# Where a sorted-token buffer gets its zero rows: first rows of every expert during attention, or behind each expert's last token

## The chip, the cores and the metric

One core of a Trainium2 chip runs the whole program. The metric is the device time of one execution in microseconds (us). The kernel before takes 522.28 us, the median of three runs (520.22 to 523.31).

## The reference

Block-summary attention gives 1536 token rows of 512 values. Each row goes through one of eight experts (top-1 by a gate), and the result goes through a dense network with a squared ReLU.

```python
x = attn_out.transpose(0, 2, 1, 3).reshape(1536, 512)
logits = x @ w_gate + modality_bias[modality_id]
e_idx = np.argmax(logits, axis=1)          # one of 8 experts per token
...
for e in range(8):
    mask = e_idx == e
    if not mask.any(): continue
    h = np.maximum(x[mask] @ w1[e], 0.0)       # 512 -> 1024
    out[mask] = gate_w[mask, None] * (h @ w2[e])   # 1024 -> 512
...
h = np.maximum(out @ w_in, 0.0)            # 512 -> 2048
return h * h @ w_out                       # 2048 -> 512
```

## The kernel before, in words

The work has three stages. **Attention** runs in NB = 12 steps of P = 128 tokens. SP loads the queries and values of each step, POOL builds the keys, TensorE (PE) computes scores, transposes and values, ACT the exponentials, DVE maxima and normalisation. The result of a step stands in `X[:, i, :]`; PE then computes its gate logits, and DVE routes the tokens in the five groups of `RGROUPS`.

**Sorting** goes through DRAM. `xs_d` has 128 rows at its start and behind them a section of EROWS = 1536 rows for each of the E = 8 experts. POOL scatters token rows into it with indirect DMAs (`scatter(g)`, L785 to L790): the token with rank r of expert e goes to row 128 + EROWS e + r. How many tokens an expert has (`cnt`) is known when the last group is routed (L925).

**Experts** are computed in tiles of 128 rows that are read back from `xs_d` into two buffers `x_in`. An expert's last tile is its last 128 rows, so it overlaps the tile before, but an expert with fewer than 128 tokens has a tile that reaches beyond its last token. Those rows must hold finite numbers, and zeros are put there. The kernel does it before the counts are known: from step i = ZFIRST = 5 of SP's load loop (L465 to L475) one DMA of 256 KB fills rows 0 to 127 of `xs_d`, and four DMAs of 512 KB fill the first 128 rows of two sections each, 2.36 MB in five DMAs on SP's queue. POOL waits for all five (L804) before the first scatter, which may overwrite them.

The most common expert so far is chosen early, and the first tiles are its: tiles 0 and 1 are loaded by POOL (L809 to L811), tile 2 by SP (L496). For tile 3 and on the rows come out of a table that DVE works out from the counts (L1142 to L1199, the last write is T_ROW, semaphore `rows`). SP waits for `rows` (L497) and then for x_t (a transpose that frees the buffer) and issues `load_x(3)` and `load_x(4)` (L486 to L488); each loads a register from the table in SBUF, computes the address and issues a DMA. On PE the order is written out: layer 1 of tile 2, the first six eighths of layer 2 of tile 1, the transposes of tile 3 (L1600, L1492), the rest of layer 2. PE runs its instructions in order, so it stands still if tile 3 has not landed. DVE's order is written out too: the last weight split (L1136), lsub (L1140), the tables, `x_low(2)` (L1168), which layer 1 of tile 2 waits for, more tables, `h_low(1)`, which layer 2 of tile 1 waits for.

Weights of the second expert come in two 2 MB DMAs that POOL issues (L849): the first after the semaphore `slots` (L1167), the second once tile 3 has landed (L867). `Seq` (L357, here `r`) is a helper on DVE: each instruction raises a semaphore and the next one waits for it.

After the experts comes the **dense network**, in which PE has dense work from L1653 to L1670.

Of the kernel before, what the change touches and what calls it, by code (L numbers as in the profile page):

```python
# [5 lines left out]
F32 = mybir.dt.float32  # L6
# [4 lines left out]
ALU = mybir.AluOpType  # L11
# [3 lines left out]
P = 128  # L15
# [7 lines left out]
NBS = S // P  # L23
# [12 lines left out]
N, DM, E, FE = B * S, H * D, 8, 1024  # L36
KD = DM // P
KF = FE // P
SPEC = 3
TILES = (N + E * (P - 1)) // P + SPEC - 1  # L40
EROWS = N
LEAST = N // P
RECENT = 4
WE = KD * FE
# [19 lines left out]
T_NR = T_DONE + 1  # L64
T_E0 = T_NR + 1
T_X0 = T_E0 + 1
T_ALL = T_X0 + SPEC

AHEAD = 1
VPITCH = 9 * P  # L70
# [6 lines left out]
TRI = 4  # L77
SPLIT_AHEAD = PARTS - 1
EARLY = 1
ZFIRST, ZSTEP = NBS - 1, 2  # L80
FRAC = 16


# [16 lines left out]
def constants():  # L100
# [4 lines left out]
    def put(a, table, name, v):  # L105
        lo, hi = table[name]
        a[:, lo:hi] = v
# [5 lines left out]
    put(f, CF, "tile_row", P * np.arange(TILES + 1)[None])  # L113
    put(f, CF, "base", (EROWS * np.arange(E) + P)[None])
    put(f, CF, "run", np.arange(E)[None])
# [7 lines left out]
    first = np.zeros((P, E), np.float32)  # L123
    first[0] = EROWS * np.arange(E) + P
    assert (first == first.astype(np.dtype("bfloat16"))).all()
# [19 lines left out]
def build(nc, a):  # L145

    base = (nc.sbuf_base + 63) // 64 * 64
# [5 lines left out]
    def sb(region, name, shape, dt):  # L153
        n = size[dt] * int(np.prod(shape[1:]))
        n = (n + 31) // 32 * 32
        t = nc.alloc_sbuf_tensor_at(name, shape, dt, offset=cursor[region])
        cursor[region] += n
        assert cursor[region] <= end[region], (name, cursor[region] - end[region])
        return t
# [5 lines left out]
    sorted_m = sb("c", "sorted_m", [P, NB + GT, 2], F32)  # L165
    table = sb("c", "table", [P, T_ALL], I32)
    waited = sb("c", "waited", [P, 4], F32)
# [3 lines left out]
    zero = sb("c", "zero", [P, DM], F32)  # L171
# [49 lines left out]
    spec_c = sb("t", "spec_c", [P, 2], F32)  # L221
    least = sb("t", "least", [P, E], F32)
    skip = sb("t", "skip", [P, E], F32)
    tiles = sb("t", "tiles", [P, E], F32)
    real = sb("t", "real", [P, E], F32)
    begin = sb("t", "begin", [P, 3, E + 1], F32)
# [20 lines left out]
    cnt = sb("t", "cnt", [P, E], F32)  # L247
# [51 lines left out]

    xs_d = nc.dram_tensor("xs_d", (P + E * EROWS, DM), F32).ap()  # L300
    ys_d = nc.dram_tensor("ys_d", (N + P, DM), F32).ap()
    meta_d = nc.dram_tensor("meta_d", (N, 2), F32).ap()

    def cfv(name):
        lo, hi = CF[name]
        at = CF["thr"][0]
        return cr[:, lo - at:hi - at]
# [5 lines left out]
    def wide(ap, axis, n):  # L313

        u = ap.unsqueeze(axis)
        shape = list(u.shape)
        shape[axis] = n
        return u.broadcast_to(shape)

    def Wv(slot, lo, col, n):  # L320
# [7 lines left out]
    names = """const const_r ident w_gate mbias cleared zero ones bias_ok logit rk  # L328
        ksum kw sc mx ex tr0 tr1 pt0 pt1 pv norm xt xtc lg rank oneh rowd vtsum sums vm vsum
        meta metas sorted rows placed slots rout oh tab n_run e0 x0 warm early lsub scat_b scat_c scat_d x2  # L330
        raw0 raw1 zfill scat_a x_t x_h x_l l1 relu ht hh hl l2 y sh sla slbv slbp
        counts both ylast wo_h wo_v zin scale zt zh zl m1 r sqs s_h s_l mo o_a o_v out ofree den_ok""".split()
    sem = {n: nc.alloc_semaphore("s_" + n) for n in names}
    s_q = [nc.alloc_semaphore(f"s_q{s}") for s in range(RING)]
# [5 lines left out]
    s_x0 = [nc.alloc_semaphore(f"s_x0_{t}") for t in range(2)]  # L340
# [72 lines left out]
    with block:  # L413

        @block.sync
        def _(sp):
            def load_q(i):
                if i >= RING:
                    sp.wait_ge(sem["sc"], i - RING + 1)
                sp.dma_start(q_in[i % RING][:, :, :], a["q"][i]).then_inc(s_q[i % RING], 16)  # L420

            def load_v(i):
                if i >= VRING:
                    sp.wait_ge(sem["pv"], i - VRING + 1)
                sp.dma_start(v_in[i % VRING][NSUM:KEYS, :, :, :].rearrange("p a h d -> p (a h d)"), a["v"][i, :, 0:2 * H * (D + 1)]).then_inc(s_v[i % VRING], 16)
# [16 lines left out]
            def load_weights(e, part):  # L442
                for n in (part, part + 1):
                    w, k = (w1_v, KD // PARTS) if n < PARTS else (w2_v, KF // PARTS)
                    j = n % PARTS
                    sp.dma_start(raw[:, n * PW:(n + 1) * PW].rearrange("p (k f) -> p k f", k=k),
                                 w[bass.ds(e, 1), :, j * k:(j + 1) * k, :].rearrange("a p k f -> (a p) k f")
                                 ).then_inc(s_raw0[n], 16)
# [16 lines left out]
            for i in range(VRING, NB):  # L465
                load_v(i)
                if i + RING < NB:
                    load_q(i + RING)
                if i == ZFIRST:
                    sp.wait_ge(sem["zero"], 1)  # L470
                    sp.dma_start(xs_d[0:P, :], zero[:, :]).then_inc(sem["zfill"], 16)
                if ZFIRST <= i < ZFIRST + E // ZSTEP:
                    some = slice((i - ZFIRST) * ZSTEP, (i - ZFIRST + 1) * ZSTEP)
                    sp.dma_start(xs_d[P:, :].rearrange("(e r) d -> r e d", e=E)[0:P, some], wide(zero[:, :], 1, ZSTEP)
                                 ).then_inc(sem["zfill"], 16)  # L475
                if i == NB - RING:
                    sp.wait_ge(sem["e0"], 1)
                    e = sp.value_load(table[0:1, T_E0:T_E0 + 1], min_val=0, max_val=E - 1)
                    load_weights(e, 0)
# [6 lines left out]
            def load_x(t, s):  # L486
                row = sp.value_load(table[0:1, bass.ds(t + T_ROW, 1)], min_val=0, max_val=E * EROWS)
                sp.dma_start(x_in[s][:, :], xs_d[bass.ds(row, P), :]).then_inc(s_xs[s], 16)  # L488
# [3 lines left out]
            sp.wait_ge(sem["x2"], 1)  # L492
            row = sp.value_load(table[0:1, T_X0 + 2:T_X0 + 3], min_val=0, max_val=E * EROWS)
            sp.wait_ge(sem["scat_d"], RGROUPS[4][1] * 16)
            sp.wait_ge(sem["x_t"], 1)
            sp.dma_start(x_in[0][:, :], xs_d[bass.ds(row, P), :]).then_inc(s_xs[0], 16)  # L496
            sp.wait_ge(sem["rows"], 1)  # L497

            def moe_step(t, s):
                sp.wait_ge(sem["x_t"], t)  # L500
                load_x(t + 1, 1 - s)
# [5 lines left out]
            with sp.Fori(0, (TILES - SPEC) // 2) as m:  # L507
                t = m * 2 + SPEC
# [242 lines left out]
        def _(pool):  # L751
# [33 lines left out]
            def scatter(g):  # L785

                pool.wait_ge(sem["rowd"], g + 1)
                for i in range(RGROUPS[g][0], sum(RGROUPS[g])):
                    pool.indirect_dma_start(out=xs_d, out_offset=bass.IndirectOffsetOnAxis(ap=dest[:, i:i + 1], axis=0),
                                            in_=X[:, i, :], in_offset=None).then_inc(sem["scat_" + "aabcd"[g]], 16)  # L790
# [10 lines left out]
            sums_of(NBS + 2)  # L801
            sums_of(NBS + 3)

            pool.wait_ge(sem["zfill"], (1 + E // ZSTEP) * 16)  # L804
            scatter(0)
            scatter(1)
            pool.wait_ge(sem["scat_a"], sum(RGROUPS[SETTLED - 1]) * 16)
            pool.wait_ge(sem["x0"], 1)
            for t in range(2):  # L809
                row = pool.value_load(table[0:1, T_X0 + t:T_X0 + t + 1], min_val=0, max_val=(E - 1) * EROWS + 2 * P)  # L810
                pool.dma_start(x_in[t][:, :], xs_d[bass.ds(row, P), :]).then_inc(s_x0[t], 16)  # L811
# [89 lines left out]
        def _(dve):  # L901
# [74 lines left out]
            r = Seq(dve, sem["rout"])  # L976
# [160 lines left out]

            dve.tensor_tensor(lsub[:, :, :], logit[:, :, :], wide(lmax[:, :], 2, E), ALU.subtract).then_inc(sem["lsub"], 1)  # L1140
            T1 = TILES + 1
            r(dve.tensor_scalar(used[:, :], cnt[:, :], 0.0, None, ALU.is_gt))  # L1142
# [157 lines left out]
            with dve.Fori(0, (TILES - SPEC) // 2) as m:  # L1300
                t = m * 2 + SPEC
# [18 lines left out]
            with dve.Fori(0, GROUPS) as g:  # L1320
                for f in range(KFF):
                    n = g * KFF + f
# [401 lines left out]
```

## Time and profile before

| What | Value |
|---|---|
| Median of three runs | 522.28 us |
| The profiled execution's own time | 521.77 us |
| Its span, first to last instruction | 520.1 us |
| PE busy (matmul) | 508.1 us, 98% of the span |
| PE weight load busy | 410.0 us, 79% |
| DVE, ACT, POOL busy | 225.4, 188.0, 87.1 us |
| Granted TensorE clock | 0.998 of full speed |
| DMA | 54.92 MB, mean 106 GB/s |

The 1.67 us between span and own time lie outside the instructions. The DMA engines are used unevenly: nearly fully over the first 52 us, in bursts of weights up to about 250 us, and hardly after.

### The profile page before, as it was taken

Reading aid. Unit: us, or ns where it says so; the run is one execution under the profiler, and the core shown is the slowest. Engines: PE = TensorE matmul, PEld = TensorE weight load, DVE = VectorE, ACT = ScalarE, POOL = GpSimd, SP = SyncE. Lnnn points to the kernel's source line nnn. Section 1 sums busy time; section 2 is a strip of 40 time slices with the busy share of each in tenths; the row PEclk is TensorE's granted clock in tenths of the full one; section 3 lists DMA queues with packets and bytes.
Section 4 is the critical chain, followed back from the end, with each engine's and each line's share of the span. In section 5 each row is a group of like instructions: output and inputs, shape, how many; then the busy total and the mean of one; then the engine's idle time right before and its main releaser. Section 6 shows DMA issues by size and latency. Waiting matters only on the chain.

```text
span 520.1 us, 9415 instructions
## 1 busy us (share of the span) xinstructions
PE 508.1 (98%) x3115; PEld 410.0 (79%) x3117; DVE 225.4 (43%) x440; ACT 188.0 (36%) x355; POOL 87.1 (17%) x110
## 2 busy tenths in 40 slices
PE   8889999999999999999999999999999999999995
PEld 3678788888888888888788888888888888888884
DVE  4787686974323554237632422342242233222221
ACT  1876665243524544225522212331221233122121
POOL 4434335027600223100000000300000020000002
PEclk9999999999999999999999999999999999999999
DMA  8999666384661655521200000400000020000002
GB/s 285 336 290 340 235 220 228 99 285 104 189 216 41 219 204 202 202 82 40 83 1 1 0 1 0 161 0 0 0 0 0 0 81 0 0 0 0 0 0 81
DMA packets 19018, 54.92 MB, mean 106 GB/s; under 512 B 2848, under 2 KB 3120, under 8 KB 18480
## 3 DMA queue, kind: packets, MB, share of 16 engines
q1 hardware_dynamic: 11200, 27.47, 16.6%
q0 software_dynamic: 5200, 23.62, 12.6%
q10 hardware_dynamic: 2592, 3.49, 1.8%
q8 instruction: 15, 0.25, 0.2%
q14 instruction: 11, 0.09, 0.1%
HBM read 42.51 MB, written 12.07 MB: 105 GB/s over the span
## 4 chain that ended last, share of the span: by engine, by line
PE 95%; DVE 3%; issue 1%; ACT 1%; POOL 0%; POOLq 0%; DVEq 0%; ACTq 0%
PE psum L1653 9%; PE psum L1654 9%; PE psum L1652 9%; PE psum L1668 8%; PE psum L1669 8%; PE psum L1670 8%; PE psum L1536 5%; PE psum L1559 5%; PE psum L1538 5%; PE psum L1560 5%; PE psum L1561 5%; PE psum L1537 5%; PE psum L1396 2%; PE psum L1569 2%; PE psum L1371 2%; PE psum L1456 2%
## 5 line engine op out<-in xcount | busy, mean ns | idle before, releaser
L1326 DVE TENSOR_TENSOR sq<-r_sb 128x512 f32<-128x512 f32 x48 | 33.2, 692 | 141.4 <-ACT r_sb L734 137.4
L734 ACT ACTIVATE r_sb<-psum 128x512 f32<-128x512 f32 x48 | 28.7, 597 | 143.7 <-PE psum L1654 143.7
L1668 PE MATMUL psum<-W,s_hi 128*128 128x512 f32 x192 | 75.9, 395 | 0.1
L1653 PE MATMUL psum<-z_lo,W 128*128 128x512 f32 x192 | 75.8, 395 | 0.0
L1654 PE MATMUL psum<-z_hi,W 128*128 128x512 f32 x192 | 75.8, 395 | 0.0
L1652 PE MATMUL psum<-z_hi,W 128*128 128x512 f32 x192 | 75.8, 395 | 0.0
L1669 PE MATMUL psum<-W,s_hi 128*128 128x512 f32 x192 | 75.5, 393 | 0.0
L1670 PE MATMUL psum<-W,s_lo 128*128 128x512 f32 x192 | 75.4, 393 | 0.0
L893 POOL DMA_INDIRECT out<-o_sb,sorted_m x12 | 11.6, 969 | 293.5 <-DVE o_sb L1342 291.6
L1328 DVE TENSOR_TENSOR s_lo<-sq,s_hi 128x512 fp32r<-128x512 f32 x48 | 33.2, 692 | 33.5 <-ACT s_hi L736 33.5
L736 ACT ACTIVATE s_hi<-sq 128x512 fp32r<-128x512 f32 x48 | 30.3, 632 | 41.8 <-DVE sq L1326 41.8
L1668 PEld LDWEIGHTS psum<-W,s_hi 128*128 128x128 f32 x192 | 36.1, 188 | 8.7 <-issue 0.5
L1652 PEld LDWEIGHTS psum<-z_hi,W 128*128 128x128 f32 x192 | 36.0, 188 | 8.7
L1654 PEld LDWEIGHTS psum<-z_hi,W 128*128 128x128 f32 x192 | 36.0, 187 | 8.7
L1653 PEld LDWEIGHTS psum<-z_lo,W 128*128 128x128 f32 x192 | 36.0, 188 | 8.6
L1670 PEld LDWEIGHTS psum<-W,s_lo 128*128 128x128 f32 x192 | 36.1, 188 | 8.2
L1669 PEld LDWEIGHTS psum<-W,s_hi 128*128 128x128 f32 x192 | 36.1, 188 | 8.1
L1536 PE MATMUL psum<-W,x_hi 128*128 (+1 forms) x104 | 42.1, 405 | 0.3 <-DVE x_lo L1018 0.3
L1559 PE MATMUL psum<-W,h_hi 128*128 (+1 forms) x104 | 42.0, 404 | 0.0
L1538 PE MATMUL psum<-W,x_lo 128*128 (+1 forms) x104 | 40.9, 393 | 0.0
L1560 PE MATMUL psum<-W,h_hi 128*128 (+1 forms) x104 | 40.9, 393 | 0.0
L1561 PE MATMUL psum<-W,h_lo 128*128 (+1 forms) x104 | 40.7, 391 | 0.0
(205 smaller groups left out, 729.5 us busy)
## 6 DMA issues: line engine op xcount, KB each, us to landing
raw<-in_w POOLq DMA_DIRECT2D x4, 2048.0 KB, 9.1
raw<-in_w_io POOLq DMA_DIRECT2D x4, 2048.0 KB, 8.2
v_in<-in_v SPq DMA_DIRECT2D x12, 390.0 KB, 12.7
raw<-in_w SPq DMA_DIRECT2D x8, 512.0 KB, 4.3
kT<-in_kT SPq DMA_DIRECT2D x8, 400.0 KB, 7.9
q_in<-in_q SPq DMA_DIRECT2D x12, 256.0 KB, 8.8
X<-in_vT SPq DMA_DIRECT2D x4, 768.0 KB, 11.7
x_in<-xs_d SPq DMA_DIRECT2D x12, 256.0 KB, 2.8
```

The costliest lines, as they stand in the source:

```text
L1326: dve.tensor_tensor(sq[:, :], r_sb[:, :], r_sb[:, :], ALU.mult).then_inc(sem["sqs"], 1)
L1536: pe.matmul(bank[h][:, :], x_hi[:, k, :], wh, start=(k == 0), stop=False)
L1538: ins = pe.matmul(bank[h][:, :], x_lo[:, k, :], wh, start=False, stop=(k == KD - 1))
L1559: pe.matmul(bank[4][:, :], h_of(t)[1][:, k, :], wh, start=(k == 0), stop=False)
L1560: pe.matmul(bank[4][:, :], h_of(t)[1][:, k, :], wl, start=False, stop=False)
L1561: ins = pe.matmul(bank[4][:, :], h_lo[:, k, :], wh, start=False, stop=(k == KF - 1))
L1652: pe.matmul(bank[f % 2][:, :], wh, z_hi[:, k, :], start=(k == 0), stop=False)
L1653: pe.matmul(bank[f % 2][:, :], wh, z_lo[:, k, :], start=False, stop=False)
L1654: ins = pe.matmul(bank[f % 2][:, :], wl, z_hi[:, k, :], start=False, stop=(k == KD - 1))
L1668: pe.matmul(bank[2 + j][:, :], s_hi[f % SBUFS][:, tok], wh, start=(f == 0), stop=False)
L1669: pe.matmul(bank[2 + j][:, :], s_hi[f % SBUFS][:, tok], wl, start=False, stop=False)
L1670: ins = pe.matmul(bank[2 + j][:, :], s_lo[f % SBUFS][:, tok], wh, start=False, stop=(f == KFF - 1))
```

## The change

The five zero DMAs become one (rows 0 to 127 only). A section grows by 128 rows, EROWS = 1664, so that each has 128 spare rows at its end. DVE computes, once `cnt` is there, one row per expert into new table entries: the row behind its last token if it has fewer than 128 tokens, and otherwise the spare rows. SP loads each of the eight into a register and issues eight DMAs of 256 KB (2.10 MB) there; then it waits for their completion before it goes on to `load_x(3)`. POOL's wait for the zero DMA (now 16, not 80) moves from before scatter(0) to behind scatter(1).

```diff
-EROWS = N
+EROWS = N + P
@@ tables
-T_ALL = T_X0 + SPEC
+T_PAD = T_X0 + SPEC
+T_ALL = T_PAD + E
-ZFIRST, ZSTEP = NBS - 1, 2
+ZFIRST = NBS - 1
@@ SP, load loop
                 if i == ZFIRST:
                     sp.wait_ge(sem["zero"], 1)
                     sp.dma_start(xs_d[0:P, :], zero[:, :]).then_inc(sem["zfill"], 16)
-                if ZFIRST <= i < ZFIRST + E // ZSTEP:
-                    some = slice((i - ZFIRST) * ZSTEP, (i - ZFIRST + 1) * ZSTEP)
-                    sp.dma_start(xs_d[P:, :].rearrange("(e r) d -> r e d", e=E)[0:P, some], wide(zero[:, :], 1, ZSTEP)
-                                 ).then_inc(sem["zfill"], 16)
@@ SP, behind the load of tile 2
             sp.dma_start(x_in[0][:, :], xs_d[bass.ds(row, P), :]).then_inc(s_xs[0], 16)
+            sp.wait_ge(sem["pads"], 1)
+            for t in range(2):
+                sp.wait_ge(s_x0[t], 16)
+            for n in range(E):
+                pad = sp.value_load(table[0:1, T_PAD + n:T_PAD + n + 1], min_val=P, max_val=E * EROWS)
+                sp.dma_start(xs_d[bass.ds(pad, P), :], zero[:, :]).then_inc(sem["zpad"], 16)
             sp.wait_ge(sem["rows"], 1)
+            sp.wait_ge(sem["zpad"], E * 16)
@@ POOL
-            pool.wait_ge(sem["zfill"], (1 + E // ZSTEP) * 16)
             scatter(0)
             scatter(1)
+            pool.wait_ge(sem["zfill"], 16)
             pool.wait_ge(sem["scat_a"], sum(RGROUPS[SETTLED - 1]) * 16)
@@ DVE, before lsub (L1140)
+            r(dve.tensor_scalar(pad_f[:, 0, :], cnt[:, :], float(P), float(N), ALU.is_ge, ALU.mult))
+            r(dve.tensor_tensor(pad_f[:, 1, :], pad_f[:, 0, :], cnt[:, :], ALU.max))
+            dve.tensor_tensor(table[:, T_PAD:T_PAD + E], pad_f[:, 1, :], cfv("base"), ALU.add).then_inc(sem["pads"], 1)
             dve.tensor_tensor(lsub[:, :, :], logit[:, :, :], wide(lmax[:, :], 2, E), ALU.subtract).then_inc(sem["lsub"], 1)
```

## Rows read from the trace of the kernel before

**Rows 1.** The page: busy time of each engine (share, instructions); chain that ended last.

```profile
PE 508.1 (98%) x3115; PEld 410.0 (79%) x3117; DVE 225.4 (43%) x440; ACT 188.0 (36%) x355; POOL 87.1 (17%) x110
...
PE 95%; DVE 3%; issue 1%; ACT 1%; POOL 0%; POOLq 0%; DVEq 0%; ACTq 0%
```

**Rows 2.** SP's timeline: start us, us, engine, line, operation, tiles; attention.

```profile
31.09 0.43 SPq L471 DMA_DIRECT2D xs_d<-zero  x1
...
47.66 0.43 SPq L474 DMA_DIRECT2D xs_d<-zero  x1
```

**Rows 3.** Stretches of attention: length, busy (instructions) per engine, PEclk, DMA share, GB/s.

```profile
38.00:47.00 9.00, 8.84 (x152) 7.52 (x151) 5.79 (x16) 6.41 (x20) 1.29 (x3) 1.00 1.03 374
47.00:52.00 5.00, 5.00 (x98) 4.10 (x87) 4.29 (x14) 3.59 (x11) 4.68 (x6) 1.00 0.87 283
```

**Rows 4.** PE's timeline, attention; in brackets the idle time before and its releaser.

```profile
36.07 1.03 PE L1396 MATMUL psum<-v_in,pT 120*64 120x65 f32 x26
38.16 0.39 PE L1396 MATMUL psum<-v_in,pT 120*64 120x65 f32 x6 [1.06 <-issue]
```

**Rows 5.** DMA queues, 35-36 us (two), 38-39 us: packets, MB, share.

```profile
q1 hardware_dynamic: 75, 0.24, 94.8%
q8 instruction: 1, 0.02, 7.9%
...
q1 hardware_dynamic: 179, 0.37, 103.1%
```

**Rows 6.** POOL's timeline, the first scatter.

```profile
53.02 1.17 POOL L789 DMA_INDIRECT xs_d<-X,dest  x1 [1.34 <-DMA xs_d<-zero]
```

**Rows 7.** DVE's timeline from the last weight split to the row table.

```profile
93.25 0.25 DVE L1140 TENSOR_TENSOR lsub<-logit,lmax 128x96 f32<-128x96 f32 x1
...
97.64 0.17 DVE L1167 CAST table<-exp_f 128x8 int32<-128x8 f32 x1
97.72 0.68 DVE L1018 TENSOR_TENSOR x_lo<-psum,x_hi 128x512 fp32r<-128x512 f32 x1
...
98.92 0.17 DVE L1173 TENSOR_SCALAR beyond<-cnt 128x8 f32<-128x8 f32 x1
99.12 0.17 DVE L1174 TENSOR_TENSOR per_e<-beyond,cr 128x8 f32<-128x8 f32 x1
...
103.31 0.18 DVE L1199 CAST table<-row_t 128x22 int32<-128x22 f32 x1
```

**Rows 8.** PE's timeline: layer 1 of tile 2, weight loads of tile 3's transposes.

```profile
98.46 0.50 PE L1536 MATMUL psum<-W,x_hi 128*128 128x512 f32 x1
...
108.40 0.42 PEld L1492 LDWEIGHTS psum<-ident,x_in 128*128 128x128 f32 x4 [0.31 <-DMA x_in<-xs_d]
```

**Rows 9.** SP's timeline: the loads of tiles 3 and 4.

```profile
104.24 0.35 SPq L488 DMA_DIRECT2D x_in<-xs_d  x1
...
105.37 0.34 SPq L488 DMA_DIRECT2D x_in<-xs_d  x1
```

**Rows 10.** DMA issues: size, us to landing; last row 100 to 109 us.

```profile
raw<-in_w POOLq DMA_DIRECT2D x4, 2048.0 KB, 9.1
...
x_in<-xs_d SPq DMA_DIRECT2D x12, 256.0 KB, 2.8
...
ys_d<-y_last SPq DMA_DIRECT2D x1, 256.0 KB, 2.1
...
x_in<-xs_d SPq DMA_DIRECT2D x2, 256.0 KB, 4.1
```

**Rows 11.** Landing time of the last zero write, issued at 47.66 us.

```profile
DMA to landing us min/median/max: 5.1/5.1/5.1
```

**Rows 12.** POOL's and ACT's timeline: second expert's weights loaded and first used.

```profile
99.13 0.81 POOL L849 DMA_DIRECT2D raw<-in_w  x1 [4.08 <-issue]
...
114.48 3.90 ACT L585 ACTIVATE W<-raw 128x1024 fp32r<-128x1024 f32 x4 [2.47 <-DVE y_sb L1179]
```

**Rows 13.** A stretch beside this load, columns as in rows 3.

```profile
104.00:105.00 1.00, 1.00 (x6) 0.74 (x5) 0.96 (x4) 0.00 (x0) 0.00 (x0) 1.00 1.06 438
```

More of the change, by code:

```diff
@@ L223, in build @@
     skip = sb("t", "skip", [P, E], F32)
+    pad_f = sb("t", "pad_f", [P, 2, E], F32)
     tiles = sb("t", "tiles", [P, E], F32)
@@ L330, in build @@
         meta metas sorted rows placed slots rout oh tab n_run e0 x0 warm early lsub scat_b scat_c scat_d x2
-        raw0 raw1 zfill scat_a x_t x_h x_l l1 relu ht hh hl l2 y sh sla slbv slbp
+        raw0 raw1 zfill pads zpad scat_a x_t x_h x_l l1 relu ht hh hl l2 y sh sla slbv slbp
         counts both ylast wo_h wo_v zin scale zt zh zl m1 r sqs s_h s_l mo o_a o_v out ofree den_ok""".split()
```

## The prediction

> **What bounds the kernel now.** I read the page first: PE is busy for 98% of the span and makes 95% of the chain that ended last [rows 1]. So two things alone can move the time: PE idle time that goes away, and PE idle time that is new. I then looked at the two places that the change touches. The first is attention, where the zero writes are issued from 31.09 to 47.66 us [rows 2]. From 38 to 47 us the DMA engines are saturated (share 1.03, 374 GB/s), which looks like a bottleneck, but PE is busy for 8.84 of 9.00 us there, and for 5.00 of 5.00 us from 47 to 52 [rows 3]. The reader is to see that a full DMA column beside a full PE column says that nobody waits for the DMAs. The second place is the start of the expert stage, 93 to 109 us, read engine by engine in time order. There PE's only idle time is 0.31 us at 108.40, before the transposes of tile 3, and the releaser is the load of `x_in` [rows 8]. That small row matters most: the load of tile 3 has no slack at all now, and the change puts four waits and eight DMAs in front of it on SP.
>
> **Part 1, zero writes leave attention.** Removed are four DMAs of 512 KB, 2.10 MB, at some 370 GB/s 5.7 us of DMA time [rows 3]. Who waits for them? POOL alone: 1.34 us before the first scatter at 53.02 [rows 6]. What it waited for on PE's side comes much later (tile 0), and scatter 1 waits for DVE's routing of its group (L787) whenever scatter 0 starts; so this gives PE nothing. The one PE idle time nearby is 1.06 us from 37.10 on (36.07 + 1.03) [rows 4]. It is inside a run of 32 like matmuls (after 26), so no semaphore ends it. Could the zero writes cause it? At 35 to 36 us SP's queue moves 75 packets for 0.24 MB, 3.2 KB each; at 38 to 39 us 179 for 0.37 MB, 2.07 KB each, the size of one row of `xs_d` [rows 5]. The queue is worked off in order, so the zeros issued at 31.09 seem to flow from about 37.5 only, behind a backlog of values and keys that stays. I take 0 us of gain, with 1.06 us as the bound; a loss is excluded as nothing is added in this stage. SP is past five issues of about 0.43 us earlier (now one), and the loads queued behind them come earlier, but PE waits for none of these.
>
> **Part 2, three small DVE instructions before lsub.** Two are chained by `r`, whose period for 8 elements is 0.20 us (98.92 to 99.12), the third is followed by an instruction that doesn't wait for it, 0.08 us (97.64 to 97.72) [rows 7]. Sum 0.20 + 0.20 + 0.08 = 0.48 us. What is behind it on DVE: `x_low(2)` ends at 97.72 + 0.68 = 98.40 and layer 1 of tile 2 starts at 98.46 [rows 7, 8]. There is no cover worth the name, so PE moves by 0.4 to 0.5 us, and the row table (end 103.31 + 0.18 = 103.49) by the same.
>
> **Part 3, eight pads on SP.** The pad rows are in the table at 93.25 + 0.20 + 0.20 + 0.17 = 93.82 us [rows 7]. SP is free by then, as tile 2, which PE uses ahead of tile 3, has been issued, and the waits on tiles 0 and 1 are long fulfilled. How long from the release to a DMA with an address from the table? The row table ends at 103.49 and load_x(3) starts at 104.24, 0.75 us. How long is the period? load_x(3) to load_x(4), the same sequence plus a wait that is already fulfilled, 105.37 - 104.24 = 1.13 us [rows 9]. So the first pad is issued at 94.57 and the eighth at 94.57 + 7 x 1.13 = 102.5 us. The first six have the DMA engines nearly to themselves: 0.26 MB each 1.13 us is 232 GB/s, against 370 and more shown [rows 3]. The last two meet the weights, which POOL issues at 99.13 (now 99.6) and which fill the engines at 104 (438 GB/s) [rows 12, 13]. Landing of a 256 KB write: 2.1 us with nothing beside it; of a 256 KB load beside the weights 4.1 us, where the median of all takes 2.8 [rows 10], so 1.3 us for the company, and 2.1 + 1.3 = 3.4 us for the last pad: 105.9 us. The other bound is the last 512 KB zero write, 5.1 us [rows 11]. I take 3.4, the same size and the same company.
>
> Then SP wakes (the wait on `rows`, 103.97, is already behind it), loads the register and issues load_x(3) at 105.9 + 0.75 = 106.65 us, 2.4 us later than 104.24. Its landing should be shorter than 4.1 us: 2.1 MB of weights, issued at 99.6 and flowing from about a microsecond later, plus the two late pads (0.5 MB) end about 107.5 at 0.39 MB/us (between the 374 of rows 3 and the 438 GB/s of rows 13), just as its data start. I take 3.3 us, between 2.8 and 4.1. So tile 3 lands at 109.95 and the transposes start at 110.0 instead of 108.40, **+1.6 us**. The 0.48 us of DVE don't add to it: both are waits of the same PE stream, and PE comes to this place at 108.4 - 0.3 + 0.48 = 108.6 and stands for another 1.4 us. Nothing behind it gives the time back, as PE runs on without idle time. Bounds: with 2.1 us for the last pad (104.6) and 2.8 for the load, tile 3 lands at 108.15 and only DVE's 0.5 us are left. With 5.1 us for the pad (107.6), 0.75 and 4.1, it lands at 112.45: +4.1 us.
>
> **Who waits behind it.** The second half of the weights is issued by POOL when tile 3 has landed (L867) and is then 1.6 us later. The first half lands at 99.13 + 9.1 = 108.2 and, with 0.48 us of DVE and 0.5 MB of pads at 0.39 MB/us ahead of it, 1.8 us later, at 110.0; its first user is ACT at 114.48 [rows 10, 12]. That is 4.5 us of cover, so it costs nothing; without the cover it would be up to 1.8 us more.
>
> A rule of the Trainium skill bears on part 3: "DMA: Bandwidth & Descriptors", section "Anatomy of one DMA — SWDGE (gpsimd) path", says that a DMA costs a fixed 2.0 us plus its bytes at 436 GB/s, most of the fixed part being the receipt of the write, longest where the target is HBM; every pad is such a write, and SP waits for its receipt. By that rule an estimate for 256 KB is 2.6 us, the last pad would land at 105.1 and the loss be 0.8 us; the trace has 2.1 us for such a write in quiet, so the rule is roughly borne out, but it has no term for the weights beside it.
>
> **The rivals.**
> (a) *The pads are hidden*: they land before the row table and only DVE's instructions are paid. For it: SP has 10 us between 93.8 and 103.97, and 2.1 MB need only 5.7. Against it: the issue period of 1.13 us, not the bandwidth, sets the pace. +0.5 us, 522.8. Chance 0.17.
> (b) *The weights hold the pads up*: slower by over 0.5%. From about 100.8 us on the last two or three pads share the engines with 2 MB, and the completion that SP waits for comes late. It decides from the point at which tile 3 lands after 111.0 us, that is when the last pad takes over 4.5 us or the period over 1.27 us. At the upper bound +4.1 us, 526.4. For it: 438 GB/s at 104 us. Against: the last pad is small. Chance 0.22.
> (c) *Attention gains*: the stall of 1.06 us is gone as the DMA queues are less full, and the zeros were in its way after all. For it: it falls 6 us after the first zero issue, with the engines saturated, and one 16 KB packet of the instruction queue at 35 us [rows 5] shows that instructions come by DMA too. Against it: the packet sizes. 1.6 - 1.06 = +0.5 us, 522.8; with the pads hidden too 0.5 - 1.06 = -0.6, 521.7. Chance 0.15; a gain of over 2.6 us needs more idle time than attention shows after 31 us, and I give it 0.05 of its own.
> The page "Runtime: NRT & Kernel Launch", section "Instruction fetch mechanics", of the Trainium skill speaks for (c): a sequencer fetches its next 256 instructions with a DMA of its own while it works on the current ones. It calls the cost mostly hidden; the row of 1.06 us shows one that probably isn't.
>
> **How the numbers follow.** The forecast, +1.6 us, has 0.41: 521.77 + 1.6 = 523.4 for the profiled execution (span 521.7), and 0.51 us more for the median, 522.28 + 1.6 = 523.9. The range reaches from (c) with hidden pads, 521.7, to (b), 526.4; the three runs lie 2 us below and 1 us above their median, so I take 520.4 to 526.9. A measurement of this kernel tells 0.5%, 2.6 us, from no change. Slower by that: (b), 0.22, and 0.03 of the forecast's upper part, 0.25. Faster: 0.05. Within: 0.70.
>
> **What would show it.** DVE: x_lo of tile 2 about 0.48 us later against the last weight split. SP: eight zero writes from about 1.3 us after that split, 1.13 us apart; if they are under 0.9 apart, (a). PE: an idle time before L1492 of tile 3 of about 1.4 us, released by `x_in`; over 2.5 us is (b), none is (a). Attention: the 1.06 us stall is there as before, else (c). DMA from 40 to 52 us is well below saturation, with PE as busy as it was. I am wrong if PE's pace in attention changes outside of such a stall, or if new idle time comes anywhere else.

## The result

The changed kernel takes 532.62 us (median of four runs, 530.13 to 535.27) against 521.26 us for the kernel before (520.22 to 523.31): a ratio of 1.0191, 95% interval 1.0147 to 1.0235 (the two medians alone would give 1.0218). It is slower by 10 to 11 us, where +1.6 us was forecast.

The page of the changed kernel: busy times, granted clock in 40 slices, chain that ended last; the busy times and the chain of before are in [rows 1].

```profile
span 533.6 us, 9463 instructions
...
PE 513.9 (96%) x3116; PEld 411.8 (77%) x3117; DVE 226.1 (42%) x443; ACT 187.9 (35%) x355; POOL 86.9 (16%) x110
...
PEclk9998999999999999999999999999999999999999
...
PE 85%; DMA 7%; DVE 2%; SPq 2%; issue 1%; POOLq 0%; POOL 0%; ACT 0%; ACTq 0%
```

PE's share of the chain fell from 95% to 85% and DMA has entered it with 7%. But PE's busy time also rose, from 508.1 to 513.9 us, for the same matmuls: not all of the loss is waiting. The span is 13.5 us longer. A convenient ruler is the start of the transposes of each tile on PE (L1492 before, L1500 after), which cuts the span in parts that can be compared between kernels.

PE's timeline of the changed kernel: transposes of tiles 2, 3 and 4.

```profile
100.23 0.60 PE L1500 MATMUL psum<-ident,x_in 128*128 128x128 f32 x4
...
118.20 0.74 PE L1500 MATMUL psum<-ident,x_in 128*128 128x128 f32 x4 [4.72 <-DMA x_in<-xs_d]
...
128.15 0.60 PE L1500 MATMUL psum<-ident,x_in 128*128 128x128 f32 x4
```

The same in the kernel before: the one of tile 3 follows its weight load at 108.40 [rows 8]; the ones of tiles 2 and 4:

```profile
95.83 0.60 PE L1492 MATMUL psum<-ident,x_in 128*128 128x128 f32 x4
...
116.68 0.60 PE L1492 MATMUL psum<-ident,x_in 128*128 128x128 f32 x4
```

| Part of the span | Before | After | Longer by |
|---|---|---|---|
| start to tile 2 | 95.83 | 100.23 | 4.4 |
| tile 2 to tile 3 | 12.58 | 17.97 | 5.4 |
| tile 3 to tile 4 | 8.27 | 9.95 | 1.7 |
| tile 4 to the end | 403.4 | 405.5 | 2.0 |

Four parts, and the prediction spoke of one. **Tile 2 to 3** is the pads. The fences that follow show SP's timeline (last pad, load of tile 3), SP's wait for the pads, and the landing times of the pads (shortest, median, longest):

```profile
107.38 0.33 SPq L500 DMA_DIRECT2D xs_d<-zero  x1
...
115.50 0.36 SPq L486 DMA_DIRECT2D x_in<-xs_d  x1
```

```profile
SPq L505 <- DMA xs_d<-zero: 7.0, 1, 7.0
```

```profile
DMA to landing us min/median/max: 2.0/2.1/7.4
```

The pads go out 1.1 us apart, as forecast, but for the last, which follows after 1.47 us. The first five land in 2.0 to 2.1 us. The last three, issued at 104.8, 105.9 and 107.4, take 6.3, 7.2 and 7.4 us. POOL issued the weights at 104.03. What the queues did from 106 to 108 us, then from 108 to 110 (q0: POOL's, q1: SP's; packets, MB, share):

```profile
q0 software_dynamic: 97, 0.40, 77.9%
q1 hardware_dynamic: 4, 0.01, 1.1%
...
q0 software_dynamic: 137, 0.56, 71.5%
q1 hardware_dynamic: 115, 0.23, 29.7%
```

SP's queue moved 4 packets from 106 to 108 us while two pads, and from 107.4 on three, had been issued and had not landed. So SP waits 7.0 us, and the load of tile 3 leaves 15.27 us after the start of tile 2's transposes (115.50 - 100.23); in the kernel before [rows 9] it was 8.41 us (104.24 - 95.83).

**Tile 3 to 4** is the clock. PE stood still for 4.72 us; right behind it (stretches of 1 us; the number before the DMA share is the granted clock):

```profile
118.00:119.00 1.00, 0.80 (x5) 0.80 (x6) 0.00 (x0) 0.02 (x1) 0.00 (x0) 0.82 0.83 221
119.00:120.00 1.00, 1.00 (x3) 0.74 (x3) 0.32 (x1) 0.58 (x1) 0.56 (x1) 0.50 0.09 33
120.00:121.00 1.00, 1.00 (x4) 0.78 (x3) 0.37 (x1) 0.00 (x0) 0.38 (x1) 0.50 0.39 41
121.00:122.00 1.00, 1.00 (x6) 0.80 (x5) 0.66 (x3) 0.00 (x0) 0.00 (x0) 0.50 0.94 274
122.00:123.00 1.00, 1.00 (x8) 0.93 (x7) 0.83 (x6) 0.69 (x2) 0.00 (x0) 0.97 1.02 180
```

From 119 to 122 us the clock is 0.50, the 1.2 GHz level, and PE, full as it looks, has 3 and then 4 matmuls in a microsecond, where it has 6 at full clock [rows 13]. The other two parts don't point at the change. **The last** has no idle time at all. **The first** is longer before any line that the change touches, and it has a stretch at the lower clock of its own, from 43.5 to 47 us, behind a stop of PE of 2.33 us; the kernel before has none in attention:

```profile
44.00:45.00 1.00, 1.00 (x7) 0.22 (x11) 0.98 (x3) 0.78 (x2) 0.00 (x0) 0.50 0.85 207
```

These two were the first thing to test.

### The profile page after: what moved, and what is told of

Read it like the earlier page. It is cut to its first block, busy times and chain, and to the rows that moved or that the text cites. A ratio compares the mean times of both kernels' runs of the same rounds, so it can differ in the third digit from the quotient of the medians.

```text
span 533.6 us, 9463 instructions
## 1 busy us (share of the span) xinstructions
PE 513.9 (96%) x3116; PEld 411.8 (77%) x3117; DVE 226.1 (42%) x443; ACT 187.9 (35%) x355; POOL 86.9 (16%) x110
## 4 chain that ended last, share of the span: by engine, by line
PE 85%; DMA 7%; DVE 2%; SPq 2%; issue 1%; POOLq 0%; POOL 0%; ACT 0%; ACTq 0%
PE psum L1661 8%; PE psum L1660 8%; PE psum L1662 8%; PE psum L1676 8%; PE psum L1677 8%; PE psum L1678 8%; DMA X<-in_vT 6%; PE psum L1567 4%; PE psum L1568 4%; PE psum L1569 4%; PE psum L1544 4%; PE psum L1545 4%; PE psum L1546 4%; PE psum L1577 2%; PE psum L1419 2%; PE psum L1404 2%
## 5 line engine op out<-in xcount | busy, mean ns | idle before, releaser
L1678 PE MATMUL psum<-W,s_lo 128*128 128x512 f32 x192 | 75.5, 393 | 0.0
L1567 PE MATMUL psum<-W,h_hi 128*128 (+1 forms) x104 | 42.8, 411 | 0.1
L1568 PE MATMUL psum<-W,h_hi 128*128 (+1 forms) x104 | 41.5, 399 | 0.0
```

Source lines behind the costliest of these rows:

```text
L1567: pe.matmul(bank[4][:, :], h_of(t)[1][:, k, :], wh, start=(k == 0), stop=False)
L1568: pe.matmul(bank[4][:, :], h_of(t)[1][:, k, :], wl, start=False, stop=False)
L1678: ins = pe.matmul(bank[2 + j][:, :], s_lo[f % SBUFS][:, tok], wh, start=False, stop=(f == KFF - 1))
```

## The experiments

**The changed kernel again, and the two halves of the change in attention.** First the unchanged "after" for a second profile; then the longer sections alone; then the missing zero writes alone; then the changed kernel with the wait on the pads behind the loads of tiles 3 and 4.

> The changed kernel again, for a second profile. In the first one three things made the loss: 4.3 us until the last weight split (input loads of attention late by 1 to 4 us, which began before any line that the change touches), 5.4 us of waiting for tile 3, 1.7 us at half clock behind it. If the attention part belongs to the change, it is there again (3 us or more). If it is the luck of one execution or of one chip, it is under 1.5 us against the kernel before on this chip, and the total loss falls to 6 to 8 us. The wait for tile 3 (4 to 6 us) should stand in both cases.

Measured: 532.47 us, ratio 1.0222 (1.0143 to 1.03). Tile 2 is at 95.38 us, 0.5 us earlier than before, so the 4.4 us of attention are gone; tile 2 to 3 is 17.79 us (+5.2), tile 3 to 4 10.65 (+2.4), the rest +2.7:

```profile
113.17 1.12 PE L1500 MATMUL psum<-ident,x_in 128*128 128x128 f32 x4 [4.55 <-DMA x_in<-xs_d]
```

The three later parts belong to the change, the first to the execution. (Of the last part, some 0.6 us is one tile step of 13.21 us with a stop of PE of 0.45 us in it, which the first profile doesn't have.) The fall of the total to 6 to 8 us that I expected with it did not come.

```diff
-EROWS = N
+EROWS = N + P
```

> The kernel before with nothing changed but the length of a section, 1664 for 1536 rows. Theory layout (longer sections move what lies in DRAM, and with it the pace of the input loads): slower by 3 to 5 us, all of it in attention, as in the changed kernel. Theory luck: within 1 us of the kernel before. Theory emptier queue (it is the missing zero writes that harm attention in some way): within 1 us as well.

Measured: 522.53 us, ratio 0.9989 (0.9958 to 1.002). Longer sections cost nothing.

```diff
@@ SP, load loop
-                if ZFIRST <= i < ZFIRST + E // ZSTEP:
-                    some = slice((i - ZFIRST) * ZSTEP, (i - ZFIRST + 1) * ZSTEP)
-                    sp.dma_start(xs_d[P:, :].rearrange(...)[0:P, some], wide(zero[:, :], 1, ZSTEP)).then_inc(sem["zfill"], 16)
+                    sp.dma_start(xs_d[P + 3 * EROWS:2 * P + 3 * EROWS, :], zero[:, :]).then_inc(sem["zfill"], 16)
@@ POOL
-            pool.wait_ge(sem["zfill"], (1 + E // ZSTEP) * 16)
+            pool.wait_ge(sem["zfill"], 2 * 16)
```

> The kernel before with one zero write of 256 KB in attention in place of the four of 512 KB (only the section that has under 128 tokens in this data; the other sections' zeros are left out), nothing else. It is the first half of the change alone. My prediction: no gain, within 1 us. Rival: the stalls of PE in attention go with the DMA traffic, 1 to 1.5 us faster. Theory emptier queue: 3 us or more slower.

Measured: 523.06 us, ratio 1.0016 (0.9991 to 1.0042). No gain, as forecast. The start of tile 0's transposes tells the same over all profiles of this study: in the ten with four zero writes in attention it lies between 71.97 and 76.59 us (mean 73.5), in the eight without between 71.80 and 76.77 (mean 74.2). Attention's length varies by 5 us from one execution to the next, whatever the kernel. What goes with it is the clock: in five of the 18 profiles (two with the four writes, three without) the granted clock is 0.50 for 3.4 us somewhere between 41 and 61 us, and these are the five latest, 75.5 to 76.8 us; the thirteen with a full clock there lie between 71.8 and 74.8 us.

```diff
             sp.wait_ge(sem["rows"], 1)
-            sp.wait_ge(sem["zpad"], E * 16)
...
             moe_step(3, 1)
+            sp.wait_ge(sem["zpad"], E * 16)
             sp.wait_ge(sem["counts"], 1)
```

> The changed kernel, but SP waits for the eight pads only after the loads of tiles 3 and 4, which in this data don't read pad rows. If the wait is what costs (7 us in the first profile: 5.4 us of waiting and 1.7 us of half clock), the kernel is 5 to 7 us faster than the changed one and the wait before tile 3 is under 1 us. Rival: it is the traffic of pads and weights itself that makes tile 3 late, as the load now stands behind the pads in the same queue; then PE still waits 3 us or more.

Measured: 529.68 us, ratio 1.011 (1.006 to 1.016), only 2.8 us faster than the changed kernel beside it; the wait of PE is 1.63 us. Neither was right: SP's wait for the pads is most of PE's stop (4.55 to 1.63 us), but not all. From tile 2 on this profile is 5.8 us shorter than that of the changed kernel, twice what the medians show; it has the low clock in attention instead, and of its four runs the one with the highest granted clock (0.997) took 527.08 us, the other three (0.994 and 0.995) 529.7 to 529.8. SP issues the load of tile 3 at 108.29, as early as it could wish, and that load itself takes 5.9 us to land, behind late pads and beside the weights. There was no half clock behind it: tile 3 to 4 took 8.36 us. And the last part was still 2.2 us longer, with neither waiting nor a low clock in front of it.

**The part without idle time.** In every profile with pads so far a tile took 12.51 us and not 12.34 (the time from one tile's transposes to the next one's). The pads' table entries are the one thing left that PE can feel: `table` is eight words longer, and all buffers behind it in SBUF move. In the kernel before they start 1216 bytes behind the region's begin, now 1248.

```diff
-T_ALL = T_X0 + SPEC
+T_PAD = T_X0 + SPEC
+T_ALL = T_PAD + E
```

> The kernel before with its table eight words longer and nothing else. In all three profiles of kernels with pads each expert tile behind tile 4 takes 12.51 us and not 12.34, and the time from tile 4 to the end is 2.0 to 2.7 us longer, with no idle time on PE; the kernels without pads don't show it. The longer table moves all buffers behind it in SBUF by 32 bytes, from 19 x 64 to 19.5 x 64 bytes. Theory addresses: this kernel shows 12.51 us as well and is 2 to 2.7 us slower than the kernel before. Rival (traffic, or later timing of the weights): 12.34 us and no loss.

Measured: 524.54 us, ratio 1.0073 (1.0038 to 1.0108). Two of its tiles in PE's timeline, then the same two of the kernel before:

```profile
141.24 0.60 PE L1493 MATMUL psum<-ident,x_in 128*128 128x128 f32 x4
153.75 0.60 PE L1493 MATMUL psum<-ident,x_in 128*128 128x128 f32 x4
```

```profile
153.98 0.60 PE L1492 MATMUL psum<-ident,x_in 128*128 128x128 f32 x4
166.32 0.60 PE L1492 MATMUL psum<-ident,x_in 128*128 128x128 f32 x4
```

12.51 us against 12.34, and tile 4 to the end +2.1 us, with no pad, no wait and not one instruction more. An unused table entry costs what looked like work.

```diff
-T_ALL = T_PAD + E
+T_ALL = T_PAD + 2 * E
```

> The changed kernel with a table that is another eight words longer, so that the buffers behind it lie at a multiple of 64 bytes again. Theory addresses: a tile takes 12.34 us, the kernel is 2 to 2.7 us faster than the changed one (about 530 us), and the wait for tile 3 of 4.5 us stays. Rival: 12.51 us, 532.5 us.

Measured: 521.66 us, ratio 1.0002 (0.998 to 1.0023), 11 us less than the changed kernel, where 2 to 2.7 were expected. The wait for tile 3 is still 4.58 us and the clock still falls; but a group of the dense network (from the transposes of its second group of 512 tokens to those of the third) takes 89.00 us, where the kernel before had 90.96. The direction was right, the size not: 1280 bytes is no return to the old place but a better one.

**The parts of the pads, at 1280 bytes.** The DVE instructions alone, put ahead of lsub in the kernel before:

```diff
+            r(dve.tensor_scalar(pad_f[:, 0, :], cnt[:, :], float(P), float(N), ALU.is_ge, ALU.mult))
+            r(dve.tensor_tensor(pad_f[:, 1, :], pad_f[:, 0, :], cnt[:, :], ALU.max))
+            dve.tensor_tensor(table[:, T_PAD:T_PAD + E], pad_f[:, 1, :], cfv("base"), ALU.add).then_inc(sem["pads"], 1)
```

> The kernel before with the three DVE instructions that compute the pad rows, buffers at a multiple of 64 bytes, no pads on SP. My prediction for this part: +0.48 us, tile 2's transposes to tile 3's 12.58 + 0.48 = 13.06 us. Rival: DVE has slack after all, 12.58 us and no loss.

Measured: 516.78 us, ratio 0.992 (0.9892 to 0.9948); tile 2 to 3 12.90 us. I had compared with the wrong place: beside the kernel before at 1280 bytes (12.42 us, below) it is exactly 0.48 us.

The changed kernel at 1280 bytes, where POOL holds the weights until the pads have landed:

```diff
             pool.wait_ge(sem["slots"], 1)
+            pool.wait_ge(sem["zpad"], E * 16)
             load_w(1, 0)
```

> The changed kernel, aligned as before, and POOL waits until the eight pads have landed before it issues the second expert's first weights. Theory weights (the last two pads stand beside the weights and so take up to 7.4 us to land): every pad lands in 2.0 to 2.2 us, PE waits under 0.7 us for tile 3, no half clock follows, 523 to 524.5 us. Rival (the issue pace of 1.1 us a pad and the register loads are what makes tile 3 late): PE still waits 2 us or more. A loss of its own would show if the weights, 4 us later, reach ACT too late.

Measured: 516.91 us, ratio 0.9927 (0.9898 to 0.9956); the 523 to 524.5 us expected were for the place at 1216 bytes. All eight pads land in 2.0 to 2.2 us, SP's wait for them is 1.7 us and PE doesn't wait for tile 3 at all; ACT waits 5.1 us for the later weights, which PE doesn't notice. Pads' landing, and SP's wait:

```profile
DMA to landing us min/median/max: 2.0/2.0/2.2
```

```profile
SPq L505 <- DMA xs_d<-zero: 1.7, 1, 1.7
```

One wait on POOL takes 4.7 us of the changed kernel away (521.66 to 516.91 us), and with it the low clock. That settles the weights as the cause of the late pads.

The kernel before at 1280 bytes, the table 16 words longer and nothing else:

```diff
-T_ALL = T_X0 + SPEC
+T_PAD = T_X0 + SPEC
+T_ALL = T_PAD + 2 * E
```

> The kernel before with its table 16 words longer, so that the buffers behind it in SBUF start at 1280 bytes (10 x 128) and not at 1216 (9.5 x 128). The kernel with the three DVE instructions at 1280 took 516.8 us, a tile 12.29 us, a group of the dense network 89.0 and not 90.97 us. Theory 128 bytes: all of this gain is the address; this kernel takes 516.4 us, and tile 2's to tile 3's transposes take 12.4 us, 0.48 us less than the 12.90 with the DVE instructions. Rival (the DVE instructions cost nothing or help in some way): 516.8 us or more, 12.9 us.

Measured: 515.49 us, ratio 0.9851 (0.9809 to 0.9892); a tile takes 12.26 us, a group 89.03, tile 2 to 3 12.42. It is faster than both kernels of this case. The whole price of the change at a good place is 521.66 - 515.49 = 6.2 us; these medians come from two chips, and from tile 2 on the two profiles differ by 7.5 us.

One pad in place of eight:

```diff
-            for n in range(E):
+            for n in (3,):
...
-            sp.wait_ge(sem["zpad"], E * 16)
+            sp.wait_ge(sem["zpad"], 16)
```

> The changed kernel at 1280 bytes with one pad in place of eight, that of the one expert with under 128 tokens (the other seven are left out). Theory weights: this pad lands in 2.1 us, long before the row table; no wait for tile 3 beyond 0.5 us, no half clock; 516.8 us, as with the DVE instructions alone. Rival (the wait or the register load on SP cost something themselves): over 518 us.

Measured: 518.72 us, ratio 0.9911 (0.9878 to 0.9944). PE doesn't wait for tile 3. The total is 1.9 us above the expected one; with 518.72 the number of the rival (over 518 us) was met, though not its mechanism: from tile 2 to tile 3 it is 13.09 us, 0.2 more than with the DVE instructions alone. The profile shows a PE wait of 1.16 us two tiles later, released by DVE's x_lo; other profiles have one of 0.2 to 0.5 us before the same line (layer 1), in one tile each. Whether its length belongs to the pad or to this execution stays open.

Seven of the eight pads cut to 16 rows:

```diff
+                if n == 3:
+                    sp.dma_start(xs_d[bass.ds(pad, P), :], zero[:, :]).then_inc(sem["zpad"], 16)
+                else:
+                    sp.dma_start(xs_d[bass.ds(pad, 16), :], zero[0:16, :]).then_inc(sem["zpad"], 16)
```

> The changed kernel at 1280 bytes; eight pads at the same pace, but seven of them (all but the one that is needed) write 16 rows and not 128, 32 KB. Theory bytes: the three pads issued after the weights are late since their 128 KB each and more get a small share beside 2 MB; with an eighth they land in 2 to 3 us and PE waits under 0.7 us for tile 3 (516.8 to 517.5 us). Rival (whatever is issued on SP's queue once the weights run is held up, however small): they land in 5 us or more and PE still waits 2.5 us or more (519 us or more).

(The "128 KB" in it should read 256 KB, the size of a pad.) Measured: 520.14 us, ratio 0.9939 (0.9909 to 0.997). The landing times of the small ones, and PE's wait for tile 3:

```profile
DMA to landing us min/median/max: 1.6/1.6/5.2
```

```profile
113.82 0.66 PE L1503 MATMUL psum<-ident,x_in 128*128 128x128 f32 x4 [2.02 <-DMA x_in<-xs_d]
```

An eighth of the bytes does not help in proportion: a write of 32 KB that takes 1.6 us alone takes up to 5.2 us beside the weights' start. PE's wait of 2.0 us lies between the two expectations, the landing time and the total are the rival's; most of the hold-up is being queued at that time, not the size. No half clock follows this stop either: tile 3 to 4 is 8.23 us.

**Which place is good, and for whom.** The kernel before with a table 32, 48 and 80 words longer (the edit is that of the experiments above, with 4 * E, 6 * E and 10 * E):

> The kernel before with its table 32 words longer: buffers behind it from 1344 bytes, 10.5 x 128, a multiple of 64 but not of 128, as 1216. Theory 128 bytes: a tile takes 12.34 us and the kernel 521 to 523 us, as before. Rival (the place of the buffers as such, or anything else at 1280): 12.29 us and 516 to 517 us.

Measured: 525.2 us, ratio 1.0036 (1.0012 to 1.0059). Neither expectation: 1344 bytes is worse than 1216.

> The kernel before with a table 48 words longer: buffers behind it from 1408 bytes, 11 x 128. At 1344 (10.5 x 128) a tile took 12.52 and a group 90.71 us, at 1216 (9.5 x 128) 12.34 and 90.97, so multiples of 64 that are none of 128 are not all alike. Theory 128 bytes: as at 1280, 12.29 us, 89.0 us, 515.5 us. Theory 256 bytes (1280 is 5 x 256, 1408 is 5.5 x 256): 12.4 us or more a tile, 90 us or more a group, 520 us or more.

Measured: 523.93 us, ratio 1.0037 (1.0005 to 1.0069). A multiple of 128 is not enough.

> The kernel before with a table 80 words longer: buffers behind it from 1536 bytes, 6 x 256. Theory 256 bytes (1280 is the one good place among 1216, 1248, 1280, 1344 and 1408, and the one multiple of 256): a tile takes 12.3 us, a group 89.0 us, the kernel 515.5 us. Rival (1280 is good for another reason): 12.4 to 12.5 us, 90.5 us or more, 521 us or more.

Measured: 515.22 us, ratio 0.987 (0.9813 to 0.9927), as the theory of 256 bytes had it.

| Buffers start at | A tile | A group of the dense network | Median |
|---|---|---|---|
| 1216 (kernel before) | 12.34 | 90.96 | 521 to 523 |
| 1248 (changed kernel's place) | 12.51 | 91.20 | 524.54 |
| 1280 = 5 x 256 | 12.26 | 89.03 | 515.49 |
| 1344 | 12.52 | 90.71 | 525.20 |
| 1408 = 11 x 128 | 12.50 | 91.07 | 523.93 |
| 1536 = 6 x 256 | 12.26 | 89.02 | 515.22 |

Then, at 1216, two sets of buffers by themselves 64 bytes further on: those of the up projection (`cursor["c"] = after_moe + 64`), and those of the down projection (`cursor["c"] = c_mark + 64` ahead of `z_in`).

> The kernel before with only the buffers z_part, z_hi and z_lo 64 bytes further on (a multiple of 128), all others where they were. The address gain at 1280 bytes has two parts, 3 x 2 us in the dense network (a group 90.97 to 89.0 us) and 0.05 us a tile. Theory z: the moving operand of the up projection sets it, a group takes 89.0 to 89.3 us and the kernel 516 to 517 us. Theory s: nothing here, 91 us. Both: about 90 us.

Measured: 517.05 us, ratio 0.99 (0.9871 to 0.9929), a group 89.37 us: theory z.

> The kernel before with only z_in, r_sb, sq, s_hi, s_lo and o_sb of the dense network 64 bytes further on. Theory s: the stationary operand of the down projection (or what ACT and DVE write for it) sets it, a group takes 89.0 to 89.3 us. Theory z: 91 us. Both: about 90 us.

Measured: 520.51 us, ratio 0.9984 (0.9959 to 1.001), a group 90.57 us. The two effects, 1.6 and 0.4 us a group, add up to the gain of 1.9 us at 1280 bytes. Matmuls from 340 to 400 us: the up projection (z) and the down projection (s) of the kernel before, then of the first of these two.

```profile
L1652 PE MATMUL psum<-z_hi,W 128*128 128x512 f32 x43 | 17.0, 395 | 0.0
L1670 PE MATMUL psum<-W,s_lo 128*128 128x512 f32 x43 | 16.9, 393 | 0.0
```

```profile
L1652 PE MATMUL psum<-z_hi,W 128*128 128x512 f32 x47 | 18.3, 389 | 0.0
L1670 PE MATMUL psum<-W,s_lo 128*128 128x512 f32 x41 | 15.9, 388 | 0.0
```

The place of the up projection's buffers decides most of it, and `z_hi` and `z_lo`, which stream through PE there, are the likely ones: 395 ns a matmul turn into 389, the same in all 47. But the down projection's third matmul gets shorter too, 393 to 388 ns, though neither of its operands was moved; why, no run here shows. In the down projection and in the expert tiles the operand that streams is `W`, which lies at one place in all runs.

## Why the prediction was wrong

**Attention: no gain.** Right: POOL's 1.34 us of waiting led nowhere, and the missing zeros alone changed nothing that can be measured. The sign named for rival (c) did come: the stall of 1.06 us is gone. A stall of PE inside like matmuls between 37 and 39 us (0.5 to 1.3 us) is in four of the ten profiles with the four zero writes and in none of the eight without. But it is missing in six of the ten as well, and attention ended no earlier without it, so it was a poor sign. The other sign, a changed pace of PE in attention, came in the first profile and belongs to the execution.

**DVE: 0.48 us.** Right: 12.42 to 12.90 us between tiles 2 and 3.

**The pace of the pads.** Nearly right: first pad 1.15 us after its row is in the table (97.97 + 0.17 to 99.29; 0.75 was forecast), then 1.08 to 1.16 us each and 1.47 for the last, 8.1 us from first to last (7.9 forecast). Where the weights are held back, the last period is 1.09 us as well.

**The landing of the last pad** is the term that failed in the sum. It was taken as 3.4 us, a quiet write of 2.1 us (it measured 2.0) plus 1.3 us "for the company", a number from a load that had been issued 5 us after the weights. The bound, 5.1 us, was from a stretch without POOL's traffic. The last three pads fall into the first microseconds of the weights, and there SP's queue all but stops: 4 packets in 2 us. The last pad took 7.4 us in the first profile, 7.1 and 7.2 in the next two. Tile 3 came 5.4 us late and not 1.6, which is 3.8 us more. The last pad's landing makes +4.0 us of it; the load's own landing, 2.7 us against the 3.3 taken, gave 0.6 back; and the last pad left 0.5 us later against tile 2 than in the sum (7.15 us behind its transposes, not 6.65). Rival (b) had this mechanism, its place and its sign, but stopped at 5.1 us and had a chance of 0.22. No row that the prediction used has a transfer issued in the first 3 us behind the weights; the nearest, the load of tile 3, was 5 us behind them.

The ends of the range don't follow from the sums that they are put down to: 521.7 less 2 us and 526.4 plus 1 us would be 519.7 and 527.4. The measured 532.62 us lies outside of those as well.

The rule that the prediction took from the Trainium skill ("DMA: Bandwidth & Descriptors", section "Anatomy of one DMA — SWDGE (gpsimd) path") is stated there for the DMAs of POOL. The pads are SP's: in quiet they landed in 2.0 to 2.1 us, where the estimate by that rule was 2.6, and the last one beside the weights took 7.4.

The page "DMA: Bandwidth & Descriptors" of the Trainium skill, section "Queues, rings and completion order", says that a DMA engine takes turns between the queues that it has work for, packet by packet. By the counts of packets the trace agrees from 108 us on, where SP's queue moves 115 to 157 packets in 2 us beside POOL's 135 to 142, but not at 106 to 108 with 4 beside 97, unless the pads were not yet at the engines then; the trace doesn't show when they got there.

**"Nothing behind it gives the time back"** was right, but nothing asked whether more would be lost behind it. The stop of PE of 4.6 to 4.7 us goes with half clock behind it, for 3.4 us of work in one profile and 4.9 in the other, 1.7 and 2.4 us of lost work. Behind the stops of 1.6 and 2.0 us before tile 3 the clock stayed at 1.00. A wait on the engine that is never idle can cost half as much again as its own length.

**The last part** was in no step, and in none of the rivals: +8 words in a table moved every buffer behind it by 32 bytes, +2.1 us behind tile 4. The change's diff showed `T_ALL = T_PAD + E`; I read it as eight integers.

The account of the changed kernel, second profile, +9.8 us: 5.2 us from tile 2 to 3 (0.5 of it DVE), 2.4 us of low clock, 2.1 us of place, 0.6 us of a tile step with a stop whose cause is open, and -0.5 us by which this execution's attention happened to be shorter.

## What to carry to other kernels

Before a transfer is moved next to another queue's burst, look at what transfers issued in the burst's first microseconds take to land, not at the quiet time plus a share; and where an engine that must not stand still waits for it, hold the burst back: one wait on POOL was worth 4.7 us here. Count a stop of PE together with the clock behind it, and look at the clock first when a stage that the change doesn't touch has another length. And look for what a change does to addresses: the cheapest gain of this case, 1.5% (0.9851), is 16 unused words that put PE's operands on a multiple of 256 bytes, and any comparison of two kernels that moves buffers measures that too.

## What the runs showed of the hardware that was not expected

- The same fp32r matmul of 128 x 512 takes 395 ns with its streaming operand at 1216 + 2048 n bytes of this region and 389 ns, without any spread, at 1280 + 2048 n; a group of the dense network goes from 90.96 to 89.03 us. 1280 and 1536 are good places; 1216, 1248, 1344 and 1408 are not, and differ between each other (a tile takes 12.34 to 12.52 us). That it is a multiple of 256 bytes counted from this region's begin fits all six; what in the memory does it, and which engine's access, was not tried.
- A write of 32 KB lands in 1.6 us alone and in up to 5.2 us when it is issued next to the start of a 2 MB load of another queue; one of 256 KB in 2.0 and 7.4 us.
- After a stop of 4.7 us PE ran at clock 0.50 for 3 us of full work (the changed kernel's first profile), after one of 4.55 us for some 5 us (its second): in the second the clock had fallen nearly 2 us before PE went on. After stops of 1.63 and 2.02 us before tile 3 it stayed at 1.00. That is no safe length: in attention, where PE stops more often, it fell in one profile (that of the moved up-projection buffers) at 42 us, behind stops of 0.8 and 0.5 us.
- The time at which attention ends varied from 71.8 to 76.8 us over 18 profiles, in kernels that don't differ there. All above 75 us have 3.4 us at clock 0.50 in attention, all below have none. The last load of values took 14.0 to 18.5 us and was mostly long where attention was long; that it causes the stops was not tried.
